# A new order of work on five engines in a chunked linear-attention kernel, with the kt transposes one group ahead

## The reference, cut to what matters

```python
for t in range(S):                      # S = 768, head_dim = 40
    y[:, :, t] = einsum('bhd,bhde->bhe', rt, state)
    Sa = einsum('bhde,bhe->bhd', state, at)
    state = state * wt[:, :, None, :] - einsum('bhd,bhe->bhde', Sa, bt) + einsum('bhd,bhe->bhde', vt, kt)
```

## Time and profile before

| | us |
|---|---|
| median of 3 runs | 1026.71 |
| the runs | 1026.48, 1026.71, 1030.57 |
| the profiled execution, its own time | 1030.51 |
| its span in the profile | 1028.5 |
| attention's steady part, pass 2 to pass 24 of TensorE | 37.31 to 344.59 from the span's start |

### The profile page before, as it was taken

One profiled execution on the slowest core, in us unless ns is written; L12 is line 12 of the kernel. 1 busy time (PEld: TensorE's weight loads), 2 busy tenths in 40 slices (PEclk: granted clock), 3 DMA queues, 4 the chain that ended last, 5 costly groups with the idle time before them and its releaser, 6 DMA issues. The chain is left out here.

```text
span 1028.5 us, 48486 instructions
## 1 busy us (share of the span) xinstructions
PE 971.7 (94%) x21468; PEld 918.8 (89%) x21468; DVE 526.6 (51%) x939; ACT 350.1 (34%) x756; POOL 301.3 (29%) x337
## 2 busy tenths in 40 slices
PE   6899999999999779899999999999999999999995
PEld 4788888888888768788999999999999999999995
DVE  4577777776777446776433344444832223322330
ACT  3456555555555423232121222232322112211220
POOL 6465555555555425912500000015700000000000
PEclk9999999999999979999999999999999999999998
DMA  7245666655676335401100000002100000000000
GB/s 246 94 163 185 184 200 207 204 176 190 195 220 208 115 98 163 136 4 45 46 1 0 0 0 0 0 0 87 55 1 20 16 4 19 19 19 0 19 19 19
DMA packets 50249, 86.80 MB, mean 84 GB/s; under 512 B 6066, under 2 KB 29746, under 8 KB 50194
## 3 DMA queue, kind: packets, MB, share of 16 engines
q1 hardware_dynamic: 48578, 81.96, 25.2%
q0 software_dynamic: 880, 3.69, 1.2%
q10 hardware_dynamic: 736, 0.48, 0.2%
HBM read 70.37 MB, written 7.86 MB: 76 GB/s over the span
## 5 line engine op out<-in xcount | busy, mean ns | idle before, releaser
L1402 ACT ACTIVATE d_h_hi<-d_bank 128x384 fp32r<-128x384 f32 x96 | 47.1, 491 | 200.1 <-PE d_bank L1484 200.1
L1439 DVE SCALAR_TENSOR_TENSOR d_h_lo<-d_bank,d_h_hi 128x384 fp32r<-128x384 f32 x96 | 53.5, 558 | 78.1 <-ACT d_h_hi L1402 78.1
L1498 PE MATMUL d_bank<-w_lo,d_h_hi 128*128 128x320 f32 x288 | 89.0, 309 | 0.0
L1498 PE MATMUL d_bank<-w_hi,d_h_lo 128*128 128x320 f32 x288 | 89.0, 309 | 0.0
L1498 PE MATMUL d_bank<-w_hi,d_h_hi 128*128 128x320 f32 x288 | 89.0, 309 | 0.0
L1402 ACT ACTIVATE c_h_hi<-c_bank 128x384 fp32r<-128x384 f32 x80 | 37.5, 489 | 145.7 <-PE c_bank L1484 145.6
L1498 PE MATMUL c_bank<-w_hi,c_h_hi 128*128 128x320 f32 x240 | 74.8, 312 | 0.0
L1498 PE MATMUL c_bank<-w_hi,c_h_lo 128*128 128x320 f32 x240 | 74.1, 309 | 0.0
L1498 PE MATMUL c_bank<-w_lo,c_h_hi 128*128 128x320 f32 x240 | 74.1, 309 | 0.0
L1451 DVE TENSOR_TENSOR d_o<-d_bank,u_all 128x320 f32<-128x320 f32 x24 | 11.8, 491 | 111.1 <-PE d_bank L1498 111.1
L1439 DVE SCALAR_TENSOR_TENSOR c_h_lo<-c_bank,c_h_hi 128x384 fp32r<-128x384 f32 x80 | 42.2, 553 | 40.2 <-ACT c_h_hi L1402 40.2
(11 more groups left out here) (264 smaller groups left out, 2840.8 us busy)
## 6 DMA issues: line engine op xcount, KB each, us to landing
e_raw<-in_e SPq DMA_DIRECT2D x72, 256.0 KB, 4.5
r_raw<-in_c SPq DMA_DIRECT2D x24, 768.0 KB
tok<-tok_of SPq DMA_DIRECT2D x24, 320.0 KB, 5.2
e_raw<-in_e SPq DMA_DIRECT2D x24, 260.5 KB, 4.3
va<-in_c SPq DMA_DIRECT2D x24, 160.0 KB, 5.1
vb<-in_c SPq DMA_DIRECT2D x24, 160.0 KB, 5.1
attention_out<-yout SPq DMA_DIRECT2D x92, 40.0 KB, 3.3
stage<-in_moe_w_ch POOLq DMA_DIRECT2D x4, 640.0 KB, 7.0
```

The costliest lines, as they stand in the source:

```text
L1402: nc.scalar.activation(h_hi[:, m, :], bank[m % 4][:, 0:TW], ACT.Relu).then_inc(h_hi_done, 1)
L1439: nc.vector.scalar_tensor_tensor(h_lo[:, m, :], bank[m % 4][:, 0:TW], 0.0, h_hi[:, m, :].bitcast(F32), ALU.max, ALU.subtract).then_inc(h_l ...
L1498: last = nc.tensor.matmul(bank[4 + t % 2][:, 0:E], lhs, rhs, start=(m == 0 and i == 0), stop=(m == NM - 1 and i == 2))
```

## The change

All five lists get a new order, and some steps another offset.

- TensorE's loop body begins at `abk` (offset -1, was the last with offset 0). `tokk` goes from between res1 and rv (offset -1) to between ut and m3 (offset 0), so it now needs `kt` one group earlier. `tokd` and `tokb` swap. `ru` goes ahead of nn0, `y_s` ahead of n2, `y_k` ahead of sol2, `y_b` from behind xsd to ahead of m1, n4 ahead of upd_k, n4t ahead of sol3, m2 ahead of rhs_v, and n8 ahead of rhs_a.
- SyncE: `e` was followed by va (-1), cp, vb, rr (-2), store; it is now followed by rr (-3) and va (-2), and store, cp and vb stand ahead of it.
- VectorE: rv goes ahead of decay. GpSimd: `kt` follows `at` directly; xs2 waits for `y`, and `at` no longer does.
- ScalarE: the copies of n4t and xsd swap, and the list begins elsewhere.
- Banks of n4, n4t, m2, n8 and ut change, and which unit waits for which semaphore changes with them.

```diff
-ORDER_SP = [("e", 0), ("va", -1), ("cp", -3), ("vb", -3), ("rr", -2), ("store", -4)]
-ORDER_DVE = [("xt", -4), ("u", -3), ("xs", -2), ("y", -4), ("m2", -2), ("n8", -2), ("suff", 0), ("aa", -1), ("ak", -1), ("decay", 0),
-             ("rv", -3), ("ru", -3), ("du2", -2), ("m1", -1)]
-ORDER_POOL = [("at", -1), ("nt0", -1), ("mt0", -1), ("bt", 0), ("kt", 0), ("t_neg", -1), ("xs2", -1)]
-ORDER_PE = [("sol0", -2), ("tokb", -1), ("tokd", -1), ("res1", -2), ("tokk", -1), ("rv", -3), ("sol1", -2), ("nn0", -1), ("ru", -3),
-            ("res2", -2), ("n2", -1), ("y_s", -3), ("sol2", -2), ("n2t", -1), ("y_k", -3), ("m1", -1), ("res3", -2), ("upd_k", -3),
-            ("upd_b", -3), ("n4", -1), ("sol3", -2), ("xsd", -2), ("y_b", -3), ("n4t", -1), ("rhs_v", -1), ("m2", -1), ("rhs_a", -1),
-            ("n8", -1), ("ut", -2), ("m3", -1), ("abk", 0)]
...
+ORDER_SP = [("store", -5), ("cp", -4), ("vb", -4), ("e", 0), ("rr", -3), ("va", -2)]
+ORDER_DVE = [("du2", -3), ("m1", -2), ("xt", -4), ("u", -3), ("xs", -2), ("y", -4), ("m2", -2), ("n8", -2), ("suff", 0), ("aa", -1),
+             ("ak", -1), ("rv", -3), ("decay", 0), ("ru", -3)]
+ORDER_POOL = [("bt", -1), ("t_neg", -2), ("xs2", -2), ("at", -1), ("kt", 0), ("nt0", -1), ("mt0", -1)]
+ORDER_PE = [("abk", -1), ("sol0", -2), ("tokd", -1), ("tokb", -1), ("res1", -2), ("rv", -3), ("sol1", -2), ("ru", -3), ("nn0", -1),
+            ("res2", -2), ("y_s", -3), ("n2", -1), ("y_k", -3), ("sol2", -2), ("n2t", -1), ("y_b", -3), ("m1", -1), ("res3", -2),
+            ("n4", -1), ("upd_k", -3), ("upd_b", -3), ("n4t", -1), ("sol3", -2), ("xsd", -2), ("m2", -1), ("rhs_v", -1), ("n8", -1),
+            ("rhs_a", -1), ("ut", -2), ("tokk", 0), ("m3", -1)]
+ORDER_ACT = [("rhs", -1), ("m3", -1), ("ut", -2), ("du0", -1), ("tokd", 0), ("tokb", 0), ("res1", -1), ("tokk", 0), ("du1", -1),
+             ("nn0", 0), ("res2", -1), ("n2", 0), ("n2t", 0), ("res3", -1), ("n4", 0), ("n4t", 0), ("xsd", -1)]
...
-PORT_AFTER = {"at": ("y", -3), "nt0": ("suff", 1), "mt0": ("decay", 1)}
+PORT_AFTER = {"nt0": ("suff", 1), "mt0": ("decay", 1), "xs2": ("y", -2)}
...
+            if name == "tokk":
+                if n == 0:
+                    pe.wait_ge(ready["kt"], 1)
+                take(n, "n8", -1)
+                for a in range(HA):
+                    last = nc.tensor.transpose(out[:, a * P:a * P + P], kt[:, 2 * a:2 * a + 2, :].rearrange("p q t -> p (q t)"), ident[:, :])
+                    took(n, a, last, ("n8", -1))
+                last.then_inc(filled["tokk"], 1)
```

More of the change, by code:

```diff
@@ L38 @@
-ORDER_ACT = [("nn0", -1), ("res2", -2), ("n2", -1), ("n2t", -1), ("res3", -2), ("n4", -1), ("xsd", -2), ("n4t", -1), ("rhs", -1),
-             ("m3", -1), ("ut", -2), ("du0", -1), ("tokb", 0), ("tokd", 0), ("res1", -1), ("tokk", 0), ("du1", -1)]
-BANKS = {"abk": (True, 0), "upd_k": (True, 1), "y_s": (True, 0), "ru": (True, 1), "rv": (True, 0), "tokd": (True, 1), "m3": (True, 1), "nn0": (False, 0), "n2": (False, 0), "n2t": (False, 1), "m1": (False, 0), "n4": (False, 0), "n4t": (False, 0), "m2": (False, 1), "n8": (False, 0), "xsd": (False, 1), "ut": (False, 1), "tokb": (False, 0), "tokk": (False, 1), "y_k": (True, 0), "y_b": (True, 0), "upd_b": (True, 1)}
@@ L42 @@
-PORT_AFTER = {"at": ("y", -3), "nt0": ("suff", 1), "mt0": ("decay", 1)}
-EMPTY = {"m3": 1, "du0": 1, "r": 2, "res1": 1, "du1": 1, "rv": 2, "res2": 1, "cp": 2, "du2": 1, "vb": 2, "res3": 1, "u": 1, "xsd": 1}
+ORDER_SP = [("store", -5), ("cp", -4), ("vb", -4), ("e", 0), ("rr", -3), ("va", -2)]
+ORDER_DVE = [("du2", -3), ("m1", -2), ("xt", -4), ("u", -3), ("xs", -2), ("y", -4), ("m2", -2), ("n8", -2), ("suff", 0), ("aa", -1),
+             ("ak", -1), ("rv", -3), ("decay", 0), ("ru", -3)]
+ORDER_POOL = [("bt", -1), ("t_neg", -2), ("xs2", -2), ("at", -1), ("kt", 0), ("nt0", -1), ("mt0", -1)]
@@ new lines @@
+ORDER_PE = [("abk", -1), ("sol0", -2), ("tokd", -1), ("tokb", -1), ("res1", -2), ("rv", -3), ("sol1", -2), ("ru", -3), ("nn0", -1),
[3 rows of a table added]
+ORDER_ACT = [("rhs", -1), ("m3", -1), ("ut", -2), ("du0", -1), ("tokd", 0), ("tokb", 0), ("res1", -1), ("tokk", 0), ("du1", -1),
+             ("nn0", 0), ("res2", -1), ("n2", 0), ("n2t", 0), ("res3", -1), ("n4", 0), ("n4t", 0), ("xsd", -1)]
+BANKS = {"abk": (True, 0), "upd_k": (True, 1), "y_s": (True, 0), "ru": (True, 1), "rv": (True, 0), "tokd": (True, 1), "m3": (True, 1), "nn0": (False, 0), "n2": (False, 0), "n2t": (False, 1), "m1": (False, 0), "n4": (False, 1), "n4t": (False, 0), "m2": (False, 0), "n8": (False, 1), "xsd": (False, 1), "ut": (False, 0), "tokb": (False, 0), "tokk": (False, 1), "y_k": (True, 0), "y_b": (True, 0), "upd_b": (True, 1)}
@@ L44 @@
+PORT_AFTER = {"nt0": ("suff", 1), "mt0": ("decay", 1), "xs2": ("y", -2)}
+EMPTY = {"m3": 1, "ut": 2, "du0": 1, "r": 2, "res1": 1, "du1": 1, "rv": 2, "cp": 2, "res2": 1, "ru": 2, "du2": 1, "vb": 2, "res3": 1, "u": 1, "xsd": 1}
 WARM = 36
@@ L133, in windows @@
                 elif empty and g + ahead < 0 and g + ahead + EMPTY.get(name, 0) >= 0:
-                    empty(name)
+                    empty(name, g + ahead)
     def passed(eng, name, groups):
@@ L237, in _, with empty @@
         unused = iter(range(32))
-        def empty(name):
+        def empty(name, n):
             k = next(unused)
@@ L370, in _, with empty @@
         unused = iter(range(32))
-        def empty(name):
+        def empty(name, n):
             k = next(unused)
+            if name == "rv":
+                passed(dve, "rv", n + 1)
             nc.vector.memset(spare[1][0:1, k:k + 1], 0.0).then_inc(ready[name], 1)
@@ L505, in unit @@
             out = bank.get(name)
+            if name == "abk":
+                take(n, "at")
+                for i, src in enumerate((bt, kt)):
+                    for a, b, par in every:
+                        c, h = (i * HA + a) * C, 2 * a + par
+                        last = mm(out[tok_half(par), b, c:c + C], src[dims(b), h, :], at[dims(b), h, :])
+                        took(n, 16 * i + 4 * a + 2 * b + par, last, "at")
+                last.then_inc(filled["abk"], 1)
             if name == "sol0":
@@ L512, in unit @@
                 last.then_inc(filled["sol0"], 1)
[L513 to L516, removed]
             if name == "tokd":
@@ L520, in unit @@
                 last.then_inc(filled["tokd"], 1)
+            if name == "tokb":
+                take(n, "ut", -2)
+                for a in range(HA):
+                    last = nc.tensor.transpose(out[:, a * P:a * P + P], bt[:, 2 * a:2 * a + 2, :].rearrange("p q t -> p (q t)"), ident[:, :])
+                    took(n, a, last, ("ut", -2))
+                last.then_inc(filled["tokb"], 1)
             if name == "res1":
@@ L529, in unit @@
                 last.then_inc(filled["res1"], 1)
[L530 to L533, removed]
             if name == "rv":
@@ L550, in unit @@
                 last.then_inc(filled["sol1"], 1)
+            if name == "ru":
+                if n == NG - 1:
+                    pe.wait_ge(ready["ut"], 2)
+                for a, b, par in every:
+                    h = 2 * a + par
+                    last = mm(out[tok_half(par), b, a * C:a * C + C], ut[dims(b), h, :], r_raw[dims(b), 0, h, :])
+                last.then_inc(filled["ru"], 1)
             if name == "nn0":
@@ L557, in unit @@
                 last.then_inc(filled["nn0"], 1)
[L558 to L564, removed]
             if name == "res2":
@@ L571, in unit @@
                 last.then_inc(filled["res2"], 1)
+            if name == "y_s":
+                take(n, "rv")
+                for a, b, par in every:
+                    q, j = tok_half(par), 2 * a + b
+                    last = mm(out[tok_half(par ^ b), b, a * D:a * D + D], r_raw[q, 2, j, :], xsd[q, j, :], a == 0, False)
+                    took(n, 4 * a + 2 * b + par, last, "rv")
             if name == "n2":
@@ L578, in unit @@
                 last.then_inc(filled["n2"], 1)
-            if name == "y_s":
-                take(n, "rv")
+            if name == "y_k":
+                take(n, "cp")
                 for a, b, par in every:
                     q, j = tok_half(par), 2 * a + b
-                    last = mm(out[tok_half(par ^ b), b, a * D:a * D + D], r_raw[q, 2, j, :], xsd[q, j, :], a == 0, False)
-                    took(n, 4 * a + 2 * b + par, last, "rv")
+                    last = mm(out[tok_half(par ^ b), b, a * D:a * D + D], rv_t[q, j, :], tok[q, 1, j, :], False, False)
+                    took(n, 4 * a + 2 * b + par, last, "cp")
+                last.then_inc(filled["y_k"], 1)
             if name == "sol2":
@@ L596, in unit @@
                 last.then_inc(filled["n2t"], 1)
-            if name == "y_k":
-                take(n, "cp")
+            if name == "y_b":
+                take(n, "ru")
                 for a, b, par in every:
                     q, j = tok_half(par), 2 * a + b
```

(54 more changed lines are left out.)

## The result

| | before | after |
|---|---|---|
| median, us | 1026.6 (4 runs, 1021.2 to 1030.6) | 1060.2 (4 runs, 1055.9 to 1063.0) |
| ratio to before | | 1.032 (95%: 1.028 to 1.035) |
| span of the profiled execution | 1028.5 | 1061.0 |

What follows compares the result with a forecast made beforehand. TensorE's own list was taken to bound the kernel (busy 293.7 of 307.3 us). With va late and at blocked, 22 passes of 15.33 us add 30 us to 1030.5; less 3.8 for the median, 1057, range 1025 to 1068.

Steps and rivals of the forecast that it cites:

- rr to rhs_v: SyncE's queue: va, behind rr's 768 KB, lands and lets rhs_v start 4.8 us after rr's issue; bounds 2.6 to 5.5.
- n8 to the end of at: VectorE and GpSimd: suff starts 1.14 us behind n8, ends at 14.24, and the blocked at ends at 15.21.
- the pass: One pass of attention's loop, abk to the next abk: 15.33 us, against 13.97 on average before.
- va behind y_k and rr: Every pass holds the chain y_k, rr, va, rhs_v; rhs_v starts at 11.37 us and TensorE waits 1.4 us there.
- The stores behind rr in the old trace: Four stores, 160 KB together, nearly through 4.8 us after rr; taken for va's landing, as the bytes are the same.
- The rival with va in time: va lands within 3.4 us of rr's issue, so rhs_v does not wait: pass 13.4 us, 1014 us; chance 0.13.
- suff ahead of at: The scan suff starts 0.09 us before at and blocks it; at ends 0.97 us after the scan.
- the single row of a drawn-out kt: Start of the old trace: kt, with a scan begun before it, takes 2.10 us for 1.18, ending 0.97 after the scan.
- What the change takes away: tokk beside ut, the loop's end in front of abk, and e ahead of rr save about 0.9 us a pass.
- kt's place on GpSimd: kt right behind at: nn0's input is there at 4.0 us, nn0 due at 4.1; counted at nothing.
- The 22 passes together: Attention's steady stretch: 22 x 15.33 = 337.3 us, against 307.3 before.
- the sum of 30 us: Whole kernel: 30 us more, from the 22 passes alone; prologue and three last passes counted at nothing.

Runs made afterwards that it cites:

- experiment 1: The changed kernel with va ahead of rr in SyncE's list: 1019.6 us, 0.993 of before.
- experiment 3: The changed kernel with va ahead of rr, and va also made to wait for y_k: 1018.0 us, 0.991 of before.
- experiment 4: The changed kernel with rr in two parts, 512 KB ahead of va and the last 256 KB behind it: 1046.2 us, 1.019 of before.
- experiment 8: The changed kernel with va ahead of rr and tokk back between res1 and rv: 1064.7 us, 1.037 of before.
- experiment 9: As experiment 8, with kt behind mt0 on GpSimd in place of ahead of nt0: 1030.9 us, 1.0025 of before.
- experiment 7: The changed kernel with va ahead of rr and TensorE's loop body turned back to end at abk: 1019.5 us, 0.993 of before.
- experiment 5: The kernel before, its own order, with only va moved behind rr in SyncE's list: 1079.8 us, 1.051 of before.
- experiment 6: The kernel before with va behind the first 512 KB of rr and ahead of its last 256 KB: 1052.1 us, 1.023 of before.
- experiment 2: The changed kernel, va still behind rr, with suff made to wait by semaphore for at: 1041.5 us, 1.014 of before.

## Why the prediction was right

Term by term, for the pass whose rows stand above (n8 to suff is part of the row below it):

| step | forecast | measured |
|---|---|---|
| abk to y_k's start | 5.74 | 5.71 |
| y_k to rr | 0.83 | 0.82 |
| rr to rhs_v | 4.8 | 4.88 |
| rhs_v to n8 | 0.49 | 0.46 |
| n8 to suff | 1.14 | 1.13 |
| n8 to the end of at | 3.35 | 3.33 |
| at to abk | 0.12 | 0.11 |
| the pass | 15.33 | 15.31 |

- **va behind y_k and rr: right**, in cause (experiments 1, 3, 4) and in when rhs_v starts. The wait itself is 1.0 us a pass by the waits' row where 1.4 was forecast, as TensorE reaches rhs_v later than was counted; va sets the moment either way. What delays it is the 768 KB in front, and not the wait for y_k alone (experiment 3). The stores behind rr in the old trace were a good stand-in for va, as they had its bytes. The rival with va in time failed on that; it is what experiments 1 and 3 then made true, and its price (1014, pass 13.4) was near their 1018 to 1020 (13.2).
- **suff ahead of at: right.** The forecast margin was 0.09 us and the measured one 0.22, because `at` started 1.35 behind n8 where 1.23 was forecast: rhs_a stood 0.38 behind n8, not 0.25. The step was called on a thin margin, and the single row of a drawn-out kt gave its price to 0.02 us. The Trainium skill (SBUF — State Buffer, Who interferes with whom) says that the one that starts first keeps the port and the other blocks; experiment 1, where the order is the other way round and the scan is the one that grows, agrees with it as to which of the two is drawn out. It is not a wait to the other's end in full: `at` ends 0.97 us behind the scan, where it takes 1.18 alone.
- **What the change takes away: right in kind.** TensorE is busy 10 us less in 21 passes, and without the two waits the pass is 13.28 on average, 0.71 less than before where some 0.9 was forecast. The usual pass is 0.47 shorter (13.22 against 13.69); the other 0.24 is that the old order's uneven passes are gone. That most of the gain is the move of tokk together with kt (experiments 8 and 9) was not foreseen; kt's place on GpSimd was counted at nothing, which holds only since tokk is early.
- **Two misses that cancel.** The passes are 15.23 on average, 0.1 less than the one worked out, which is 2 us over 21. The pass across the loop's exit is 17.4, 2.0 more than counted for it, and 2.0 is what experiment 7 took off it by letting the body end at abk. The 22 passes together: forecast 337.3, measured 337.1. Beside them the first pass was counted at its old length and is 3.2 us longer. Its granted clock is 0.86 where it was 1.00 before: TensorE runs at half clock from 33 to 41 us, behind waits of 2.9, 1.4 and 1.8 us, and is busy 2.1 us longer for the same loads. So two thirds of the 3.2 us are the clock. Every version run had a longer first pass than the old order as it was: 22.6 to 24.9 us in those of the new order, 21.7 and 22.1 in experiments 5 and 6. Why the waits there are longer was not tried. So the sum of 30 us for an unchanged rest met 32.5 in span, and the median moved by 33.6. That the 22 passes agree to 0.2 us is luck; the mechanism and the terms of a pass are not.

## What to carry to other kernels

In an in-order transfer queue, the place of a small load counts by what it waits for and by the bytes ahead of it: ask for each load which step of the same pass it is read by, and let it stand ahead of a large one that has a pass of slack. Which of two operations that share a port comes first can hang on little (0.22 us here, forecast at 0.09); order the one that nothing waits for behind the other, by a semaphore, in place of leaving it to chance. And when a list's steps are moved, follow single buffers: a step that reads one buffer late holds whatever stands behind its writer.

## What the runs showed of the hardware

- One wait of 1.9 us on average in each pass of 16.3 brought TensorE's granted clock to 0.92 over the stretch (15 of 21 passes at 0.82 to 0.90, the others at 1.00), and cost 0.5 us a pass beyond the wait. One of 1.1 us per pass of 15 left it at 1.00 (experiment 6), while waits of 1.2 to 1.3 us came before the three passes of 21 at 0.89 in experiment 2.
- The scan over two SBUF inputs takes 1.24 us alone and 2.22 beside `at`; decay's scan, which now has no GpSimd operation beside it, went from 1.76 to 1.24 us in the changed kernel.
- In two kernels most of whose steady passes repeat to 0.01 us (experiments 1 and 7) the first pass takes 23.6 us, 3 more than in the old order, and part of it runs at half clock.
